# One product in place of logit products and row transposes in the attention stage of a retention, expert and cosine-gate kernel

## The reference, cut to what matters

```python
# retention without softmax: B=4, H=8, S=576, D=64
ret = scale * (q @ k.T) * gamma ** (i - j)          # i >= j, else 0
x = (ret @ v) -> [2304, 512]                        # rows = tokens
# mixture of experts, E=8, the two best of each token
logits = x @ w_gate
noisy = logits + log1p(exp(x @ w_noise)) * noise
top2 = two largest of noisy; weights = softmax over the two
y = sum over the two of weight * (relu(x @ w1[e]) @ w2[e])
# dense layer with cosine gate
h = y @ w_in;  out = (h * cos(h)) @ w_out
```

## Time and profile before

| | |
|---|---|
| median of 3 runs | 973.49 us |
| profiled execution | 970.68 us, span 968.8 us |
| TensorE busy | 954.9 us (99%) |
| VectorE busy | 560.4 us (58%) |
| ScalarE busy | 476.7 us (49%) |
| GpSimd busy | 94.9 us (10%) |
| granted TensorE clock | 1.00 |
| chain that ended last | TensorE 82%, VectorE 6%, ScalarE 6%, issue 3%, DMA 2%, GpSimd 1% |

### The profile page before, as it was taken

How to read it: one execution, slowest core, us unless ns; L and a number is a source line. 1 busy time by engine, 2 the same in 40 slices (tenths; PEclk the granted TensorE clock), 3 DMA queues, 4 the chain that set the end, 5 groups by cost and what they waited for, 6 DMA issues and landing times.

```text
span 968.8 us, 17039 instructions
## 1 busy us (share of the span) xinstructions
PE 954.9 (99%) x6144; PEld 856.7 (88%) x6144; DVE 560.4 (58%) x1118; ACT 476.7 (49%) x889; POOL 94.9 (10%) x93
## 2 busy tenths in 40 slices
PE   8999999999999999999999999999999999999998
PEld 8988879999999999999999989888888888888987
DVE  4788645545545545534332145567777777776665
ACT  1446334335344344333332156567666765766555
POOL 2276600000000000000000132101000100000000
PEclk9999999999999999999999999999999999999999
DMA  9988456498979897873317159877675766656561
GB/s 364 346 326 300 183 193 223 157 309 313 306 254 325 283 331 253 265 255 129 132 65 271 59 168 322 275 276 257 254 261 210 265 224 235 231 204 240 220 236 55
DMA packets 79521, 231.92 MB, mean 239 GB/s; under 512 B 6880, under 2 KB 32736, under 8 KB 71264
## 3 DMA queue, kind: packets, MB, share of 16 engines
q1 hardware_dynamic: 73696, 212.20, 61.7%
q0 software_dynamic: 5760, 18.88, 5.3%
HBM read 168.14 MB, written 62.91 MB: 238 GB/s over the span
## 4 chain that ended last, share of the span: by engine, by line
PE 82%; DVE 6%; ACT 6%; issue 3%; DMA 2%; POOL 1%; SPq 0%; DVEq 0%; POOLq 0%
PE ps L1678 18%; PE ps L1696 17%; PE ps L1871 13%; PE ps L1857 11%; PE ps L1785 3%; PE ps L1797 3%; PE ps L1599 2%; PE ps L1622 2%; PE ps L1726 2%; PE ps L1650 2%; PE ps L1584 2%; PE ps L1714 2%; ACT angle L960 2%; PE ps L1614 2%; DVE angle L1449 1%
## 5 line engine op out<-in xcount | busy, mean ns | idle before, releaser
L1678 PE MATMUL ps<-xs,w_hi 128*128 (+1 forms) x784 | 182.9, 312 | 0.0
L1871 PE MATMUL ps<-w_sb,g_hi 128*128 128x512 f32 x576 | 180.4, 394 | 0.1
L1279 DVE TENSOR_TENSOR w_lo<-raw,w_hi 128x1024 fp32r<-128x1024 f32 x48 | 58.8, 1226 | 157.4 <-ACT w_hi L799 157.4
L1678 PEld LDWEIGHTS ps<-xs,w_hi 128*128 128x128 f32 x784 | 133.1, 188 | 0.7
L1678 PE MATMUL ps<-xs,w_lo 128*128 (+1 forms) x392 | 121.1, 309 | 0.0
L1857 PE MATMUL ps<-x_odd,w_sb 128*128 128x320 f32 x672 | 117.7, 310 | 2.2 <-DVE h_sb L1434 1.2
L1857 PEld LDWEIGHTS ps<-x_odd,w_sb 128*128 128x128 f32 x672 | 106.2, 188 | 14.5 <-DVE h_sb L1434 2.5
L799 ACT ACTIVATE w_hi<-raw 128x1024 fp32r<-128x1024 f32 x48 | 50.9, 1060 | 128.5 <-PE ps L1696 124.3
L1871 PE MATMUL ps<-w_sb,g_lo 128*128 128x512 f32 x288 | 112.5, 390 | 0.0
L1871 PEld LDWEIGHTS ps<-w_sb,g_hi 128*128 128x128 f32 x576 | 101.0, 188 | 9.8 <-issue 0.3
L719 POOL DMA_INDIRECT y<-y_slots,pos_i x36 | 35.5, 985 | 619.9 <-SPq L639 433.2
(11 more groups left out here) (193 smaller groups left out, 1615.4 us busy)
## 6 DMA issues: line engine op xcount, KB each, us to landing
w_sb<-w_pairs SPq DMA_DIRECT2D x24, 1792.0 KB
w_sb<-w_pairs SPq DMA_DIRECT2D x40, 1024.0 KB, 10.5
raw<-weights SPq DMA_DIRECT2D x64, 512.0 KB
w_pairs<-stage SPq DMA_DIRECT2D x24, 1024.0 KB, 6.9
y_slots<-zeros_sb SPq DMA_DIRECT2D x42, 256.0 KB, 4.1
gath<-x_slots SPq DMA_DIRECT2D x40, 256.0 KB, 6.2
y_slots<-y_sb SPq DMA_DIRECT2D x40, 256.0 KB, 2.1
qk<-qk SPq DMA_DIRECT2D x18, 512.0 KB, 6.8
```

The costliest lines, as they stand in the source:

```text
L1279: tt(w_lo[:, at], raw[:, f % 2, :], w_hi[:, at].bitcast(F32), ALU.subtract).then_inc(split_done, 1)
L1678: last_one = nc.tensor.matmul(ps[5 + half][:, 0:HALF], w[:, at:at + P], xs[:, bass.ds(g % 2, 1), a, k, half * HALF:(half + 1) * HALF].rear ...
L1871: last_one = nc.tensor.matmul(ps[j][:, :], a[:, slot % 2, part, j * C:(j + 1) * C], w2_sb[slot % 3][:, hl, part * DM:(part + 1) * DM], sta ...
```

## The change

- The four logit products and the four transposes of a tile become four products. The moving operand is 144 columns wide (`GW`): the 128 columns of the unit matrix and the 16 gate and noise columns of that block of channels, in the order unit, gates for even blocks and gates, unit for odd ones. Blocks 0 and 1 go to bank 5, blocks 2 and 3 to bank 6 (`row_bank`), placed so that the gate columns of both fall on the same 16 columns and are summed there, while the rows stand to the left and right.
- Before its products of tile t, TensorE waits for the two copies and for the logits of tile t-1.
- ScalarE copies the rows in two instructions of 2 x 128 columns. In the last step it does so before the softplus of the last group, not after.
- VectorE sums the logits of the two banks into SBUF (`sum_logits`): a copy of one bank's 16 columns, and an addition of the other's. It stands behind `decay_k(s)`, for tile s-2; for the last two tiles behind the two `x_low` of the first blocks, ahead of `place_rows(NG - 2)`.
- Softplus and first choice read the logits in SBUF. The counts are alone in bank 7, and a count waits for the ranks of the group before.
- The scatter of tile 11 waits for the rows of all tiles, where it waited for the logits. `x_done` counts two per tile.
- The host puts the unit matrix beside the gates: the load is 128 x 4 x 144 values, where it was 128 x 4 x 16.

```diff
-            wg = keep("wg", [P, KD_TILES, 2 * E], F32, st)
+            wg = keep("wg", [P, KD_TILES, GW], F32, st)
...
+        def row_bank(k):
+            return ps[5 + k // 2]
+
+        def logits_of(t, n):
+            return both_sb[:, t * 2 * E:(t + n) * 2 * E].rearrange("c (t e) -> c t e", e=2 * E)
...
# ScalarE, step(s)
                 t = s - 2
+                if 0 <= t < NT:
+                    act.wait_ge(rows_ps_done, t + 1)
+                    for k in range(0, KD_TILES, 2):
+                        nc.scalar.activation(x_sb[t][:, k * P:(k + 2) * P].rearrange("c (k d) -> c k d", d=P),
+                                             row_bank(k)[0:C, 0:2 * GW].rearrange("c (k d) -> c k d", d=GW)[:, :, 0:P],
+                                             ACT.Copy).then_inc(x_done, 1)
                 if t == NT - 1:
                     softplus(NG - 1)
-                if 0 <= t < NT:
-                    act.wait_ge(rows_ps_done, t + 1)
-                    nc.scalar.activation(x_sb[t][:, :], ps[5][0:C, :], ACT.Copy).then_inc(x_done, 1)
...
# VectorE
+            def sum_logits(t):
+                dve.wait_ge(x_done, 2 * t + 2)
+                nc.vector.tensor_copy(first_half[:, :], row_bank(0)[0:C, P:P + 2 * E]).then_inc(half_done, 1)
+                dve.wait_ge(half_done, t + 1)
+                tt(both_sb[:, t * 2 * E:(t + 1) * 2 * E], row_bank(2)[0:C, P:P + 2 * E], first_half[:, :], ALU.add
+                   ).then_inc(logit_done, 1)
...
                     decay_k(s)
+                if 0 <= s - 2 < NT - 2:
+                    sum_logits(s - 2)
...
                 x_low(0, j)
+            for t in range(NT - 2, NT):
+                sum_logits(t)
             place_rows(NG - 2)
...
# TensorE, step(s)
                     pe.wait_ge(xT_done, t + 1)
-                    at = (t - GROUPS[k_]) * 2 * E
+                    above(pe, x_done, 2 * t)
+                    above(pe, logit_done, t)
                     for k in range(KD_TILES):
-                        last_one = nc.tensor.matmul(logit_bank(k_)[0:C, at:at + 2 * E], xT[t % 2][:, k, :], wg[:, k, :],
-                                                    start=k == 0, stop=k == KD_TILES - 1)
-                    last_one.then_inc(logit_done, 1)
-                    above(pe, x_done, t)
-                    for k in range(KD_TILES):
-                        last_one = nc.tensor.transpose(ps[5][0:C, k * P:(k + 1) * P], xT[t % 2][:, k, :], ident)
+                        at = P * (k % 2)
+                        last_one = nc.tensor.matmul(row_bank(k)[0:C, at:at + GW], xT[t % 2][:, k, :], wg[:, k, :],
+                                                    start=k % 2 == 0, stop=True, skip_group_check=True)
                     last_one.then_inc(rows_ps_done, 1)
```

More of the change, by code:

```diff
@@ L52 @@
 TB = TPB * C
+GW = P + 2 * E
 SIZES = (3, 5, 5, 5)
@@ L201, in build @@
             xT = [keep(f"xT{i}", [P, KD_TILES, C], F32, st) for i in range(2)]
-            wg = keep("wg", [P, KD_TILES, 2 * E], F32, st)
-            used = -(-ATTN_W // 8) * 8 + 3 * 2 * DM + 3 * 2 * DM + 2 * DM + 2 * DM + DM // 2 + 3 * 2 * DM + 2 * DM + KD_TILES * 2 * E
+            wg = keep("wg", [P, KD_TILES, GW], F32, st)
+            used = -(-ATTN_W // 8) * 8 + 3 * 2 * DM + 3 * 2 * DM + 2 * DM + 2 * DM + DM // 2 + 3 * 2 * DM + 2 * DM + KD_TILES * GW
             keep("below_rows", [P, 2 * RING * CHUNK + TPU * DM - used], F32, st)
@@ L215, in build @@
             hots = keep("hots", [C, 2, NT * E], F32, st)
+            both_sb = keep("both_sb", [C, NT * 2 * E], F32, st)
             before_sum = grid("before_sum", (NT + 1) * E)
@@ L226, in build @@
             g_a = grid("g_a", NT)
+            first_half = grid("first_half", 2 * E)
             n_e, over, ends, off = grid("n_e", E), grid("over", E), grid("ends", E), grid("off", E)
@@ L272, in build @@
         chain, soft_chain, soft_done = sem("chain"), sem("soft_chain"), sem("soft_done")
+        half_done = sem("half_done")
         picked_done, counted, ranked, pos_done = sem("picked_done"), sem("counted"), sem("ranked"), sem("pos_done")
@@ L317, in group_of @@
             return next(k for k in range(NG) if GROUPS[k] <= t < GROUPS[k + 1])
-        def logit_bank(k):
-            return ps[7 - k % 2]
+        def row_bank(k):
+            return ps[5 + k // 2]
+        def logits_of(t, n):
+            return both_sb[:, t * 2 * E:(t + n) * 2 * E].rearrange("c (t e) -> c t e", e=2 * E)
+        COUNTS = ps[7]
         def x2_bank(n):
@@ L677, in scatter_rows @@
                 pool.wait_ge(pos_done, group_of(t) + 1)
-                pool.wait_ge(x_done, t + 1)
+                pool.wait_ge(x_done, 2 * t + 2)
                 nc.gpsimd.indirect_dma_start(
@@ L705, in _ @@
                 elif t == LATE_FROM + 2:
-                    pool.wait_ge(logit_done, NT)
+                    pool.wait_ge(rows_ps_done, NT)
                 elif t in PACED:
@@ L745, in softplus @@
                 above(act, picked_done, k)
-                z = logit_bank(k)[0:C, 0:n * 2 * E].rearrange("c (t e) -> c t e", e=2 * E)[:, :, E:2 * E]
+                z = logits_of(lo, n)[:, :, E:2 * E]
                 nc.scalar.activation(soft_a[:, 0:n * E].rearrange("c (t e) -> c t e", e=E), z, ACT.Abs
@@ L768, in step @@
                     act.wait_ge(out_done, t + 1)
-                    above(act, logit_done, t - 1)
                     above(act, rows_ps_done, t - 1)
@@ L1097, in first_choice @@
                 lo, hi, n = tiles_of(k)
-                both = logit_bank(k)[0:C, 0:n * 2 * E].rearrange("c (t e) -> c t e", e=2 * E)
+                both = logits_of(lo, n)
                 if k == 0:
@@ L1123, in place_rows @@
                 lo, hi, n = tiles_of(k)
-                bank = logit_bank(k)
+                bank = COUNTS
                 dve.wait_ge(counted, k + 1)
@@ L1565, in count @@
                 lo, hi = GROUPS[k], GROUPS[k + 1]
-                n, bank = hi - lo, logit_bank(k)
+                n, bank = hi - lo, COUNTS
                 pe.wait_ge(picked_done, k + 1)
+                above(pe, ranked, k)
                 if k == 0:
@@ L1640, in step @@
                 if 0 <= t < NT:
-                    k_ = group_of(t)
                     if t == 0:
@@ L1644, in step @@
                         pe.wait_ge(wg_in, 16)
-                    if t == GROUPS[k_]:
-                        above(pe, ranked, k_ - 1)
                     pe.wait_ge(xT_done, t + 1)
-                    at = (t - GROUPS[k_]) * 2 * E
+                    above(pe, x_done, 2 * t)
+                    above(pe, logit_done, t)
                     for k in range(KD_TILES):
-                        last_one = nc.tensor.matmul(logit_bank(k_)[0:C, at:at + 2 * E], xT[t % 2][:, k, :], wg[:, k, :],
-                                                    start=k == 0, stop=k == KD_TILES - 1)
-                    last_one.then_inc(logit_done, 1)
-                    above(pe, x_done, t)
-                    for k in range(KD_TILES):
-                        last_one = nc.tensor.transpose(ps[5][0:C, k * P:(k + 1) * P], xT[t % 2][:, k, :], ident)
+                        at = P * (k % 2)
+                        last_one = nc.tensor.matmul(row_bank(k)[0:C, at:at + GW], xT[t % 2][:, k, :], wg[:, k, :],
+                                                    start=k % 2 == 0, stop=True, skip_group_check=True)
                     last_one.then_inc(rows_ps_done, 1)
@@ L1924 @@
     rows = moe2_w_out.reshape(FP, 2, P, DM).transpose(0, 2, 1, 3).reshape(FP, P, 2 * DM)
-    gates = np.concatenate([moe_w_gate, moe_w_noise], axis=1).reshape(KD_TILES, P, 2 * E).transpose(1, 0, 2)
+    gates = np.concatenate([moe_w_gate, moe_w_noise], axis=1).reshape(KD_TILES, P, 2 * E)
+    unit = np.eye(P, dtype=np.float32)
+    gates = np.stack([np.concatenate([unit, g] if k % 2 == 0 else [g, unit], axis=1) for k, g in enumerate(gates)], axis=1)
     arrays = {
```

## The result

The changed kernel takes 978.17 us (median of 5 runs, 977.08 to 980.62), the kernel before beside it 973.49 (5 runs). The medians lie 4.7 us apart: slower. The ratio over all runs, which isn't that of the two medians (1.0048), is 1.0059, with an interval of 1.0042 to 1.0076, or 4.1 to 7.4 us. The forecast was 977.5, slower. Four runs more of it, in a later group, gave a ratio of 1.0063 (1.0039 to 1.0086).

The account below looks back on a forecast made before the run. TensorE was taken to bound the kernel, VectorE a near second; TensorE's 3.2 us saving against VectorE's sums, waits and late tail carried to +4.3 us on 973.49, shaded to 977.5 us; 8-in-10 range 971.5 to 981.5.

Parts of the forecast that it names:

- TensorE bounds, VectorE is the near second: Whole run: TensorE busy 954.9 of 968.8 us; in attention steps 10 to 17 VectorE busy 33.01 of 36.70 us.
- The product, 1.28 us: TensorE per tile: eight passes of 0.135 us plus 0.2 for start and end, 0.20 us less than before.
- rival of four times a transpose: TensorE's new product: 0.27 us a pass, TensorE paces attention, +18 us, 991 in all; chance 0.04.
- ScalarE's copies 0.67, VectorE's sum 0.37: Per tile: two row copies take 0.67 us, rows ready 0.08 later; VectorE's copy and addition add 0.37 us.
- The added wait: VectorE's in-order sum waits for ScalarE's copy, delayed by softplus: about 0.7 us each in steps 10 and 14.
- Scale(10) 1.2 earlier, scale(17) 2.1 later: VectorE's scale ends 1.2 us earlier at tile 10, 2.1 later at tile 17; VectorE paces steps 12 to 17.
- Low halves 3.1 later: End of attention: the two low halves that open the first product end 3.1 us later.
- First product +3.3, second-layer +4.3: After attention: first expert product 3.3 us later, second-layer product 4.3 us later, passed on to the end.
- First scatter near 110, read back over near 130.3: GpSimd's first scatter of tile 13 near 110 us, the blocks read back over near 130.3 us.
- From there the same lengths as before: Everything behind the read back was to last as long as before, so the shift stays 4.3 us.
- Choices read logits from SBUF in place of PSUM ... taken as nothing: VectorE's choices: changed operand source costs a few hundredths in 10 operations, counted as nothing.
- the late tail: End of attention: tile 17's product waits for tile 16's sum behind the low halves, then softplus; second-layer product 4.3 us later.

Follow-up runs that it names:

- e2: The changed kernel with the old four logit products and four transposes per tile, put into the new layout; median 978.32 us, ratio 1.0046 to the kernel before.
- e4: The changed kernel with each in-loop sum's copy and addition on VectorE done a second time into spare tiles; median 981.17 us, ratio 1.0071 to the kernel before.
- e5: The changed kernel with GpSimd's scaling of tile t's queries held until VectorE starts scale(t); median 977.34 us, ratio 1.0067 to the kernel before.
- e1: The changed kernel with VectorE's sum moved behind the step's choices and placing, ahead of the low split; median 973.93 us, ratio 1.0015 to the kernel before.
- e8: The changed kernel with unread zero matmuls, 10 before tile 17's product and 14 before the read back's transposes; median 977.62 us, ratio 1.0064 to the kernel before.
- e7: The changed kernel with the sum late in VectorE's step, tile 17's product in two other banks, GpSimd's scaling held until scale(t); 973.58 us, ratio 1.0015.
- e3: The kernel before plus only VectorE's copy, addition and their wait for ScalarE's row copy, results unused; median 975.82 us, ratio 1.0023 to the kernel before.
- e11: The kernel of e1 with 10 unread matmuls of zeros ahead of the read back's transposes; median 973.59 us, ratio 1.0004 to the kernel before.
- e9: The kernel before with 14 unread matmuls of zeros ahead of the read back's transposes; median 970.66 us, ratio 0.9989 to the kernel before.

## Why the prediction was right, point by point

- **TensorE bounds, VectorE is the near second.** Right, and the reason for all else. e2 and e4 are the two sides of it: 0.30 us more per tile on TensorE costs 0.93 us at the first product (1.45 at tile 17's product), 0.34 more per tile on VectorE costs 2.85.
- **The product, 1.28 us.** Right in kind: a pass costs about what a transpose of its width costs. Size off: 1.18 us, 8 x 0.123 + 0.2. The 0.2 for start and end was right. The pass wasn't: it was scaled from 0.12 us a transpose, which has the four transposes' start in it; they are 0.109 apart, and 0.109 x 144/128 is 0.123. The saving is 4.8 us over 16 tiles, not 3.2. The rival of four times a transpose is out.
- **ScalarE's copies 0.67, VectorE's sum 0.37.** Measured 0.66 and, with the gap between the two operations, 0.37 (the copy's start at 100.72 to the addition's end at 101.08).
- **The added wait.** Right that it costs, wrong in how it is spread: the longest were in step 6 (1.12 us), at 47.83 (1.17) and in step 17 (1.03); in step 14 it was 0.52, and in step 10 there was none, because VectorE came late itself, held by GpSimd; in e5, where it isn't, the wait in step 10 is 1.21 us. e1, which takes the sum out of the way of choices and scale, gives back 4.3 us.
- **Scale(10) 1.2 earlier, scale(17) 2.1 later.** Scale(17) starts at 92.76 us, was 90.85: 1.9, close, but by luck. Scale(10) starts at 55.72, was 55.01: 0.7 later and not 1.2 earlier, and from there to scale(17) only 1.2 us are added, where 3.3 were forecast. The early part failed in steps 6 and 7, where the wait of 1.12 us and the operation held from 39.05 us put scale(7) 1.6 us back; in e5, with nothing held, scale(10) is 1.7 us early. So VectorE sets the pace from the scores of tile 8 on and in places, not from step 12 on.
- **Low halves 3.1 later:** start 99.51, was 96.74: 2.8.
- **First product +3.3, second-layer +4.3.** +3.8 and +5.1, in the profile with the half clock, which is about 0.9 of the 3.8 (from the start of tile 17's product to the first product 1.79 us, and 0.89 in e8). Before the change the first product followed the low halves' end (98.03 us in the earlier trace rows) by 1.15 us and not by 1.3. The links are as described (sum of 16, product, copies, sum, softplus). e7, without the first of them, has both 1.5 us earlier than e1.
- **First scatter near 110, read back over near 130.3.** 110.81 and 131.85.
- **From there the same lengths as before.** Wrong for the profiled run: 1.6 us for the clock behind the pause, 2.9 behind the experts (2.7 net, from the second part's first product to the end). The medians have +4.7 in all, beside a forecast of +4.3 from the profiled execution that was set at +4.0.
- **"Choices read logits from SBUF in place of PSUM ... taken as nothing."** Wrong as a term: by this, the first operation of each choice can be held by GpSimd's, and one was, for 1.0 us more. The other 2.6 us of the three stretched operations don't come from it, as these read two SBUF tiles before the change as well (e3 has the same with the choices as they were). They come from the shift of the steps against GpSimd's, which the prediction left out when it carried the steps forward with VectorE's measured durations: in these,'s 1.03 us for `k_dec` among them, 5.2 us of holding are hidden. In the changed kernel it is 6.6. The net 1.4 us doesn't show in the total, beside TensorE's saving, which was under-sized by 1.6 us, and e5 says that part of the held time is no loss.

So the mechanism was right (VectorE's sums and their wait, and the late tail), and that the time came within 0.7 us of the forecast is in part luck: the early steps lose where they were to gain, the late ones lose less, TensorE's saving was too small and GpSimd's holding left out.

## What to carry to other kernels

When two engines are nearly level, as here, taking 0.3 us of work off the pace can be a loss if its neighbour gets 0.37 us for it, above all when the new work stands in an in-order queue behind a wait and ahead of what the pace engine needs: the first thing to try is to put it last in its step. When an operand moves from PSUM to SBUF, or VectorE's steps shift, look at what GpSimd does at that time: a duration read from a profile may already hold a wait for it. And when a run differs from its neighbour by more than the landmark does, compare the clock behind each pause before explaining it.

## What the runs showed of the hardware

- A VectorE operation with two SBUF inputs and GpSimd's scaling, which reads SBUF, don't run side by side: 0.18 us became 1.17, 1.22 became 2.71, 0.68 up to 1.49 in the kernel before, beside a 1.27 us operation; where `w_lo` started first in e5, GpSimd's 1.27 became 1.98 to 2.22. Operations that read PSUM kept their length within 0.07 us.
- An fp32 product of 144 columns for 128 rows is two passes, which start 0.123 us apart; transposes of 128 columns start 0.109 us apart, 16-column passes of the logits 0.112. Eight passes of 144 columns and eight of 16 differ by 0.18 us (1.18, and 1.00 in e2).
- TensorE's granted clock falls to its lower level (0.50, 1.2 GHz of 2.4) behind short pauses: after idle times of 0.96 and 1.01 us in the changed kernel, and after 1.93 in e7; not after 1.11 before e7's second-layer product, where it stayed at 1.00. The length of the pause alone doesn't decide it. Two kernels with the same instructions up to there, e1 and e11, one at full and one at half clock (timelines of TensorE):

```profile
96.98 1.22 PE L1673 MATMUL ps<-wg,xT 128*128 128x144 f32 x8 [1.71 <-DVE both_sb L1175]
```

```profile
96.76 2.26 PE L1673 MATMUL ps<-wg,xT 128*128 128x144 f32 x8 [1.69 <-DVE both_sb L1175]
```

Matmuls of zeros in the pause kept it at 1.00 in e8 and e9.
